# Own rows of v loaded first and averaged in place; the first expert block's second weights issued behind its gathers

## The reference, cut to what matters

```python
# attention: window of +-15 keys, plus 24 block summaries (block 32) for every query
k_sum = k.reshape(B, H, 24, 32, D).max(axis=3)
v_sum = v.reshape(B, H, 24, 32, D).mean(axis=3)
scores_l = where(|i - j| < 16, q k^T / 8, -1e9)
scores_s = q k_sum^T / 8 + log(32)
a = softmax(concat(scores_l, scores_s))
x = a @ concat(v, v_sum)                      # then rows by token: 1536 x 512
# first mixture: top 1 of 8 experts, 512 -> 1024 -> 512, relu, scaled by the gate
x[mask_e] = gate * (relu(x[mask_e] @ w1[e]) @ w2[e])
# last part: dense 512 -> 2048 -> 512, leaky relu
out = leaky(x @ w_in) @ w_out
```

## Time and profile before

| what | value |
|---|---|
| median of 3 runs | 526.29 us (523.98 to 526.91) |
| the profiled execution: its own time | 529.43 us |
| its span | 527.7 us |
| TensorE busy | 507.8 us, 96% |
| mean granted clock of TensorE | 0.988 of full |
| data moved | 69.04 MB |

### The profile page before, as it was taken

One profiled execution on the slowest core, in us unless ns is written; L12 is line 12 of the kernel. 1 busy time (PEld: TensorE's weight loads), 2 busy tenths in 40 slices (PEclk: granted clock), 3 DMA queues, 4 the chain that ended last, 5 costly groups with the idle time before them and its releaser, 6 DMA issues.

```text
span 527.7 us, 9199 instructions
## 1 busy us (share of the span) xinstructions
PE 507.8 (96%) x3231; PEld 421.5 (80%) x3232; DVE 264.9 (50%) x530; ACT 240.6 (46%) x509; POOL 102.6 (19%) x174
## 2 busy tenths in 40 slices
PE   6799998999999999999999999999999999999996
PEld 5577776998888888888788888888888888888885
DVE  2779686477235450354075157436416735723731
ACT  4678677532444450353164355325426604633510
POOL 6143502725051101101320000150000014000011
PEclk9999999699999999999999999999999999999999
DMA  9999989103939323415144411350640414040001
GB/s 195 234 220 207 228 191 379 45 0 97 342 16 302 125 93 129 142 43 194 60 160 171 151 77 52 150 199 0 239 159 0 158 62 177 3 156 0 0 20 60
DMA packets 74145, 69.04 MB, mean 131 GB/s; under 512 B 47232, under 2 KB 49280, under 8 KB 74112
## 3 DMA queue, kind: packets, MB, share of 16 engines
q1 hardware_dynamic: 64128, 54.16, 35.1%
q0 software_dynamic: 3584, 10.50, 6.2%
q10 hardware_dynamic: 6400, 3.94, 2.7%
HBM read 58.62 MB, written 9.97 MB: 130 GB/s over the span
## 4 chain that ended last, share of the span: by engine, by line
PE 77%; DVE 1%; issue 0%; POOLq 0%; ACT 0%
PE psum L1868 12%; PE psum L1870 12%; PE psum L1869 12%; PE psum L1793 12%; PE psum L1794 11%; PE psum L1795 11%; PE psum L1732 2%; PE psum L1855 1%; PE psum L1846 1%; PE psum L1847 1%; PE psum L1848 1%; PE psum L1856 1%; PE psum L1857 1%; PE psum L1835 0%; DVE hot_row L1315 0%
## 5 line engine op out<-in xcount | busy, mean ns | idle before, releaser
L1793 PE MATMUL psum<-xT_hi,w_hi 128*128 128x512 f32 (+1 forms) x288 | 111.3, 387 | 0.5 <-issue 0.5
L1794 PE MATMUL psum<-xT_lo,w_hi 128*128 128x512 f32 (+1 forms) x288 | 110.5, 384 | 0.0
L1795 PE MATMUL psum<-xT_hi,w_lo 128*128 128x512 f32 (+1 forms) x288 | 110.4, 383 | 0.0
L1868 PE MATMUL psum<-w_hi,h_hi 128*128 128x512 f32 x280 | 109.9, 393 | 0.0
L1870 PE MATMUL psum<-w_hi,h_lo 128*128 128x512 f32 x280 | 109.0, 389 | 0.0
L1869 PE MATMUL psum<-w_lo,h_hi 128*128 128x512 f32 x280 | 109.0, 389 | 0.0
L1440 DVE TENSOR_TENSOR h_full<-psum,h_small 128x512 f32<-128x512 f32 x48 | 33.2, 692 | 75.1 <-ACT h_small L959 73.6
L959 ACT ACTIVATE h_small<-psum 128x512 f32<-128x512 f32 x48 | 28.7, 598 | 88.8 <-PE psum L1795 56.0
L1793 PEld LDWEIGHTS psum<-xT_hi,w_hi 128*128 128x128 f32 x288 | 54.2, 188 | 11.0 <-issue 0.9
L1795 PEld LDWEIGHTS psum<-xT_hi,w_lo 128*128 128x128 f32 x288 | 54.2, 188 | 10.1
L1794 PEld LDWEIGHTS psum<-xT_lo,w_hi 128*128 128x128 f32 x288 | 54.2, 188 | 9.8
(11 more groups left out here) (241 smaller groups left out, 600.5 us busy)
## 6 DMA issues: line engine op xcount, KB each, us to landing
w_raw<-in_moe_w_in SPq DMA_DIRECT2D x12, 1024.0 KB
w_raw<-in_moe_w_out SPq DMA_DIRECT2D x6, 2048.0 KB
w_raw<-in_moe_w SPq DMA_DIRECT2D x6, 1024.0 KB
w_raw<-in_moe_w SPq DMA_DIRECT2D x3, 2048.0 KB
x_rows_sb<-y_rows SPq DMA_DIRECT2D x12, 256.5 KB, 7.9
q_nat<-in_q SPq DMA_DIRECT2D x12, 256.0 KB, 6.6
x_rows<-x_cur ACTq DMA_DIRECT2D x12, 256.0 KB, 4.3
vw_first<-in_v SPq DMA_DIRECT2D x10, 192.0 KB, 5.3
```

What stands on the lines that cost most here:

```text
L1793: mm(h, w1_hi[:, c, cols], xT_hi[:, c, 0:n], start=(c == 0), stop=False)
L1794: mm(h, w1_hi[:, c, cols], xT_lo[:, c, 0:n], start=False, stop=False)
L1795: last = mm(h, w1_lo[:, c, cols], xT_hi[:, c, 0:n], start=False, stop=(c == KD - 1))
L1868: mm(y_ps[s % 2], h_hi[:, c, rows], w2_hi[:, c, :], start=(c == 0), stop=False)
```

## The change

Two parts. First, each strip's partitions are laid out anew: 0 to 63 the strip's own rows (`load_own`), 64 to 87 the means, then 16 rows from above (`UP`) and 16 from below (`DOWN`), which `load_beside` fetches by themselves. Keys, mask and `pt` follow the same order. All own rows of batch 0 are asked for before anything else of v, `v_nat` and its load are gone, and `mean_first(t)` multiplies the own rows in place, strip by strip: 48 matmuls over 64 rows each where 24 over 128 were. The last tile's means come behind `scores(2)`, which moves ahead of unit 0. ScalarE's copy of the means into `vsum` goes; GpSimd copies from the first strip. GpSimd builds `avg` with 288 columns on 64 partitions (144 on 128 before) and the mask in more, smaller pieces, and waits after each `edge_k`. Second, SP waits for the three gathers of the first expert block before it issues `load_w2`.

```diff
+UP = STRIP + NSUM
+DOWN = UP + WINDOW
...
-        vsum = att("vsum", [NSUM, B, H, D])
+        vsum = att("vsum", [UP, H, D])
...
-        avg = att("avg", [P, QT, NSUM])
+        avg = att("avg", [STRIP, STRIPS, NSUM])
...
-        v_nat = att("v_nat", [P, H, QT * D])
...
-            def load_strips(t):
-
+            def load_own(t):
                 b, i = divmod(t, QT)
                 for s in (2 * i, 2 * i + 1):
-                    lo, hi = max(0, s * STRIP - WINDOW), min(S, (s + 1) * STRIP + WINDOW)
-                    part = NSUM + lo - (s * STRIP - WINDOW)
-                    sp.dma_start(vw[b][part:part + hi - lo, s, :, 0:D],
-                                 v[b, :, lo:hi, :].rearrange("h p d -> p h d")).then_inc(v_loaded[t], 16)
+                    sp.dma_start(vw[b][0:STRIP, s, :, 0:D],
+                                 v[b, :, s * STRIP:(s + 1) * STRIP, :].rearrange("h p d -> p h d")).then_inc(own_loaded[t], 16)
+
+            def load_beside(t):
+                b, i = divmod(t, QT)
+                for s in (2 * i, 2 * i + 1):
+                    for part, row in ((UP, s * STRIP - WINDOW), (DOWN, (s + 1) * STRIP)):
+                        if 0 <= row < S:
+                            sp.dma_start(vw[b][part:part + WINDOW, s, :, 0:D],
+                                         v[b, :, row:row + WINDOW, :].rearrange("h p d -> p h d")).then_inc(beside_loaded[t], 16)
...
-            load_v()
+            for t in range(QT):
+                load_own(t)
             sp.wait_ge(zeros_ready, 6)
-            load_strips(0)
+            load_beside(0)
+            load_beside(1)
             load_q(2)
             load_k(1, 0)
-            load_strips(1)
...
-                load_strips(t)
+                if t >= QT:
+                    load_own(t)
+                load_beside(t)
...
             sp.wait_ge(vsum_done, B)
+
+            for s in range(SUB0):
+                sp.wait_ge(rows_gathered[s], 16)
             load_w2(first_e)
...
-            chain(nc.gpsimd.memset(mask[:, :, :, 0:NSUM], -math.log(BLOCK)))
-            chain(nc.gpsimd.memset(mask[:, :, :, NSUM:], 0.0))
+            chain(nc.gpsimd.memset(mask[:, :, :, STRIP:UP], -math.log(BLOCK)))
+            chain(nc.gpsimd.memset(mask[:, :, :, 0:STRIP], 0.0))
+            chain(nc.gpsimd.memset(mask[:, :, :, UP:], 0.0))
...
+                for part, n, at in ((0, STRIP, 0), (UP, WINDOW, -WINDOW), (DOWN, WINDOW, STRIP)):
...
-                pool.wait_ge(vsum_copied, b + 1)
+                if b == 0:
+                    pool.wait_ge(vsum_spread, 1)
+                    pool.wait_ge(vsum_ready, 2)
+                    means = vw[0][STRIP:UP, 0, :, 0:D]
+                else:
+                    pool.wait_ge(vsum_copied, 1)
+                    means = vsum[STRIP:UP]
                 for s in (2 * i, 2 * i + 1):
-                    nc.gpsimd.tensor_copy(vw[b][0:NSUM, s, :, 0:D], vsum[:, b]).then_inc(vsum_ready, 1)
+                    nc.gpsimd.tensor_copy(vw[b][STRIP:UP, s, :, 0:D], means).then_inc(vsum_ready, 1)
...
+                pool.wait_ge(kt_edged, m - PIECES + 1)
...
-                if n == 0:
-                    act.wait_ge(vsum_ready, 2)
-                    for i in range(4):
-                        last = nc.scalar.copy(vsum[:, 0, i * MG:(i + 1) * MG], vsum_ps[i])
-                    last.then_inc(vsum_copied, 1)
...
-            def mean_first():
-                pe.wait_ge(avg_ready, 1)
-                pe.wait_ge(ksum_maxed, 2 * PAIRS)
-                pe.wait_ge(q_ready, 2)
-                for j in range(QT):
-                    pe.wait_ge(vn_loaded[j // (QT // 2)], 16)
+            def mean_first(t):
+                if t == 0:
+                    pe.wait_ge(avg_ready, 1)
+                    pe.wait_ge(ksum_maxed, 2 * PAIRS)
+                    pe.wait_ge(q_ready, 2)
+                pe.wait_ge(own_loaded[t], 32)
+                for s in (2 * t, 2 * t + 1):
                     for i in range(4):
-                        last = mm(vsum_ps[i], avg[:, j, :], v_nat[:, i * MG:(i + 1) * MG, j * D:(j + 1) * D],
-                                  start=(j == 0), stop=(j == QT - 1))
-                last.then_inc(vsum_done, 1)
+                        last = mm(vsum_ps[i], avg[:, s, :], vw[0][0:STRIP, s, i * MG:(i + 1) * MG, 0:D],
+                                  start=(s == 0), stop=(s == STRIPS - 1))
+                if t == QT - 1:
+                    last.then_inc(vsum_done, 1)
...
-                    pe.wait_ge(v_loaded[t], 32)
+                    pe.wait_ge(own_loaded[t], 32)
+                    pe.wait_ge(beside_loaded[t], 48 if i in (0, QT - 1) else 64)
...
             scores(1)
-            mean_first()
+            for t in range(QT - 1):
+                mean_first(t)
+            scores(2)
+            mean_first(QT - 1)
...
-                if n + 2 < UNITS:
+                if 0 < n < UNITS - 2:
                     scores(n + 2)
```

More of the change, by code:

```diff
@@ L279, in build @@
         k_loaded = [[sem(f"k_loaded{b}{half}") for half in range(2)] for b in range(B)]
-        vn_loaded = [sem(f"vn_loaded{half}") for half in range(2)]
+        own_loaded = [sem(f"own_loaded{t}") for t in range(T)]
         v_rows_loaded = sem("v_rows_loaded")
         q_loaded = [sem(f"q_loaded{t}") for t in range(T)]
-        v_loaded = [sem(f"v_loaded{t}") for t in range(T)]
+        beside_loaded = [sem(f"beside_loaded{t}") for t in range(T)]
         gate_loaded = sem("gate_loaded")
@@ L402, in load_k @@
                     sp.dma_start(k_nat[b][:, half, j], k[b, :, rows, :].rearrange("h p d -> p h d")).then_inc(k_loaded[b][half], 16)
[L404 to L408, removed]
             def load_v_rows():
@@ L551, in _ @@
-            chain(nc.gpsimd.memset(mask[:, :, :, 0:NSUM], -math.log(BLOCK)))
-            chain(nc.gpsimd.memset(mask[:, :, :, NSUM:], 0.0))
+                                    pattern=[[-STRIP, STRIPS], [BLOCK, NSUM]], channel_multiplier=-1).then_inc(avg_ready, 1)
+            chain(nc.gpsimd.memset(mask[:, :, :, STRIP:UP], -math.log(BLOCK)))
+            chain(nc.gpsimd.memset(mask[:, :, :, 0:STRIP], 0.0))
+            chain(nc.gpsimd.memset(mask[:, :, :, UP:], 0.0))
             for s in range(2):
[L555 to L559, removed]
@@ L560, in _ @@
-            chain(nc.gpsimd.memset(mask[0:64, 0, :, NSUM:NSUM + WINDOW], -NEG))
-            nc.gpsimd.memset(mask[64:128, 2, :, COLS - WINDOW:], -NEG).then_inc(mask_ready, 1)
+                for part, n, at in ((0, STRIP, 0), (UP, WINDOW, -WINDOW), (DOWN, WINDOW, STRIP)):
+                    band = mask[64 * s:64 * s + 64, :, :, part:part + n].rearrange("p k r c -> p (k r) c")
+                    if part != DOWN:
+                        chain(nc.gpsimd.affine_select(out=band, in_=band, compare_op=ALU.is_ge, fill=-NEG, base=at + WINDOW - 1,
+                                                      pattern=[[0, 3 * HG // 2], [1, n]], channel_multiplier=-1))
+                    if part != UP:
+                        chain(nc.gpsimd.affine_select(out=band, in_=band, compare_op=ALU.is_ge, fill=-NEG, base=WINDOW - 1 - at,
+                                                      pattern=[[0, 3 * HG // 2], [-1, n]], channel_multiplier=1))
@@ L563, in _ @@
+            chain(nc.gpsimd.memset(mask[0:64, 0, :, UP:DOWN], -NEG))
+            nc.gpsimd.memset(mask[64:128, 2, :, DOWN:], -NEG).then_inc(mask_ready, 1)
             pool.wait_ge(mask_ready, 1)
@@ L845, in copy_kt @@
                 s = half * n
-                body = NSUM + WINDOW
-                last = nc.scalar.copy(whole[:, s:s + n, body:body + STRIP], mine)
+                last = nc.scalar.copy(whole[:, s:s + n, 0:STRIP], mine)
                 up = n - half
@@ L850, in copy_kt @@
                 if b == 0:
-                    nc.scalar.copy(whole[:, s + 1:s + 1 + up, NSUM:body], mine[:, 0:up, STRIP - WINDOW:])
-                    last = nc.scalar.copy(whole[:, s - 1 + skip:s - 1 + n, body + STRIP:], mine[:, skip:, 0:WINDOW])
+                    nc.scalar.copy(whole[:, s + 1:s + 1 + up, UP:DOWN], mine[:, 0:up, STRIP - WINDOW:])
+                    last = nc.scalar.copy(whole[:, s - 1 + skip:s - 1 + n, DOWN:], mine[:, skip:, 0:WINDOW])
                 last.then_inc(kt_copied, 1)
@@ L922, in _ @@
             for s in range(2):
-                last = nc.scalar.copy(vw[0][0:NSUM, s, 3 * MG:4 * MG, 0:D], vsum_ps[3])
+                last = nc.scalar.copy(vw[0][STRIP:UP, s, 3 * MG:4 * MG, 0:D], vsum_ps[3])
             last.then_inc(vsum_spread, 1)
@@ L1166, in spread_first, with copy_vsum @@
                 for i in range(3):
[L1167 removed]
+                    last = nc.vector.tensor_copy(vw[0][STRIP:UP, 0:2, i * MG:(i + 1) * MG, 0:D],
                                                  vsum_ps[i].unsqueeze(1).to_broadcast([NSUM, 2, MG, D]))
                 last.then_inc(vsum_ready, 2)
[L1171 to L1172 removed]
+            def copy_vsum():
+                dve.wait_ge(vsum_done, B)
```

(1 more changed line is left out.)

32 lines of the change are left out of this document (14 added, 18 removed).

## The result

**Slower: 533.15 us against 525.19** (medians of 4 runs each on one chip), ratio 1.0143, 95% interval 1.0112 to 1.0174. The forecast was 527.0 with a range to 530.1, so it was wrong, by 6 us. The profiled execution of the changed kernel took 533.16 us, 3.7 more than that of before (529.43).

A forecast was written before the change was run, and what follows sets the result against it. PE, busy 507.8 of 527.7 us, was taken as the bound. The profiled 529.43 us plus 0.7 from the front and 0 from part 2 gave 530.1; the median, 3.14 lower in the runs, was forecast at 527.0, range 522.4 to 530.1.

The forecast's parts named there:

- What bounds the kernel, and that a delay at unit 3 is carried on: PE, busy 507.8 of 527.7 us, bounds; a delay at unit 3 reaches the end of attention unchanged.
- The front: "they move at 209 and 230 GB/s; the last own rows land at 19.7": Batch 0's v in 256-byte pieces at those rates: last own rows land 2.0 us after 17.7.
- The bound of 2.5 us: Upper bound on how much later than 17.7 us batch 0's last own rows land; lower bound 0.
- The rival of the small loads: Seven 32 KB loads before k take 5.6 us to issue and starve the queue; k at 27.9, 528.5 us; chance 0.11.
- k of batch 1 at 26.4, waited for: k, behind v in the queue, lands after PE is ready (25.9); transpose_k(8) starts at 26.4, 1.2 us later.
- Unit 0's output at 22.0, unit 3 at +0.7: Start of attention: unit 0's output 1.8 us later than 20.19; unit 3 0.7 us late, bounds -0.5 and +1.5.
- The slower rival, the clock in the front: PE's waits for own rows and k lower its clock for 8.6 us: +3 on top of 0.7, 530.0 us; chance 0.14.
- a wait of 1.97 us before 14.18 did not bring it down: Evidence against a clock fall in the front: an early PE wait in the profile left the clock up.
- Part 2, "cost 0; without that cover, 1 us": Second weights, issued after the gathers, land at 100.7; ScalarE reads at 104.79, slack 4 us; undisturbed, 1 us late.
- The faster rival, the disturbance at 88 us: w2 traffic made softmax(23) 2.14 us late; part 2 removes that: -4.3 net, 522.7 us; chance 0.16.
- The rest of part 1 at nothing: GpSimd's preparation (about 1.5 us more), its copies, edge_k's eight extra waits and smaller strips cost or gain 0.
- The 0.5 us of tile 1's strips: PE's wait before unit 2's output, attributed to tile 1's second strip, goes: 0.5 us gained.

The follow-up runs named there:

- pieces_128: Kernel before, with v_nat loaded in six loads of 256-byte pieces on 128 partitions instead of two loads of 768-byte pieces; ratio 1.0049.
- halves_768: Kernel before, with v_nat in four loads to 64 partitions each, pieces still 768 bytes; ratio 1.0038.
- means_apart: Changed kernel without SP's wait for gathers, batch 0's means again from v_nat loaded ahead, own rows fetched tile by tile; 532.57 us, ratio 1.0071.
- short_fill: Changed kernel plus three unused identity matmuls behind the means of each of tiles 1 to 4, in PE's waits for own rows; 532.22 us, ratio 1.0116.
- whole_again: The changed kernel unaltered, run again on another occasion beside a variant with filler matmuls; 533.64 us, ratio 1.0151 to the kernel before.
- mended_change: Changed kernel without SP's wait for gathers, plus three identity matmuls behind the means of tiles 1 to 4 and four in unit 22; 533.15 us, ratio 1.0061.
- earlier_v_fill: Kernel before with v_nat in 1536-byte pieces, means head by head, v_rows one tile earlier, four identity matmuls in unit 22; 530.18 us, ratio 1.0019.
- fill_both: Kernel before with v_rows one tile earlier, four identity matmuls in unit 22 and two in the wait for v_nat; 532.73 us, ratio 1.0043.
- part 2 alone: Kernel before with only SP's wait for the three gathers added ahead of load_w2; 529.22 us, ratio 0.9992.
- earlier_v: Kernel before with v_nat in 1536-byte pieces (two loads of four heads), means head by head, v_rows one tile earlier; 535.08 us, ratio 1.0096.
- front_filled: Changed kernel without SP's wait for gathers, plus eight unused identity matmuls in each PE wait for own rows of tiles 2 to 5; 540.47 us, ratio 1.0199.

## Why the prediction was wrong

- **What bounds the kernel, and that a delay at unit 3 is carried on**: right. The 30 us from 58 on are as full as before.
- **The front: "they move at 209 and 230 GB/s; the last own rows land at 19.7"**: this step failed. 154 GB/s, last means at 24.24. The bound of 2.5 us was worked out from loads to 96 and 128 partitions and said nothing of 64; pieces_128 shows that it about held for those (2.6 us), and halves_768 that loads to 64 partitions cost as much with large pieces (3.2 us).
- **The rival of the small loads**: it did not come. They were issued at 0.43 us and up, seven in 4.45 us by the timeline of SP, and nothing waited for them. By the Trainium skill's DMA: Bandwidth & Descriptors (the table under Bandwidth) they would have been the trouble; this case doesn't bear that out.
- **k of batch 1 at 26.4, waited for**: its term fell with the one before. transpose_k(8) ran at 32.12 without a wait; the means had become the later of the two. In means_apart, where they were not, k was the wait, 2.32 us.
- **Unit 0's output at 22.0, unit 3 at +0.7**: 27.01 and +6.4. Of that 4.8 us are late data by short_fill, and the rest the clock (2.9 us in whole_again, which came to +7.8).
- **The slower rival, the clock in the front**: the mechanism came, for +3 as priced, but on top of 4.8 and not of 0.7. Its chance, 0.14, rested on "a wait of 1.97 us before 14.18 did not bring it down". In mended_change the clock fell right behind that very wait, and so it did in pieces_128, earlier_v_fill and fill_both (their 32 matmuls there take 1.51 to 1.59 us). One execution in which it did not was weak evidence.
- **Part 2, "cost 0; without that cover, 1 us"**: right alone (0.9992), and its condition was named. The size without the cover was wrong: w2 was taken to land 7.5 us after its issue, and took 10.1 (9.5 in part 2 alone). So in the changed kernel ScalarE waited 2.89 us and PE 2.13.
- **The faster rival, the disturbance at 88 us**: the disturbance did go, and the time did not fall, since PE's wait for `chosen` took its place. The cause named for it, the traffic of w2, falls: part 2 alone had the wait without that traffic. Whether part 2 takes it away where part 1 is there too stays open; the traces of such kernels would fit that.
- **The rest of part 1 at nothing** (GpSimd's preparation, the waits in edge_k): no wait of PE on them shows. The 0.5 us of tile 1's strips did go.

What stays open: what "remote" is; what lowers the clock in one execution and not in the next of the same kernel; which part of the 154 GB/s is the 64 partitions, the size of the loads and the layout they go to; and how the residual 0.7% of means_apart splits between the extra 64-partition loads, the small ones and the clock.

## What to carry to other kernels

Before a load is moved to the front of a queue, take its rate from a load of the same shape, partitions, size and target included: pieces of 256 bytes came at 218 GB/s in loads of 256 KB to 128 partitions, and at 154 in loads of 128 KB to one half. A second copy of data in a shape that loads fast can be cheaper than one copy that serves both uses. A term that rests on one execution's clock, or on a cover that is itself an accident of one execution (a stall, a low clock), belongs in the range with its price without the cover.

## What the runs showed of the hardware

- Loads to 64 partitions, half as large as those to 128, which the forecast had priced as any others: 200 GB/s where 128 partitions had 302, for pieces of 768 bytes; 189 with the halves in turn where 128 had 218, for 256 bytes; 154 to 157 for own rows, on one half only. The 1536-byte pieces of earlier_v moved at 309 GB/s over 12 to 18 us.
- 2 MB behind an idle queue took 9.5 to 10.3 us to land, with a store of x and a gather beside it; the 384 GB/s of the earlier trace rows would make it 5.5.
- The granted clock behind the same instructions differed from one execution to the next, as early as 15 us. It stayed at 0.50 from 16 to 30 us in mended_change and rose by 23 us in front_filled, both with PE busy throughout.
- Four matmuls in PE's wait of about 2 us at the end of attention went with a clock of 1.00 behind it in four traces; without them it was low in all eight that had this wait.
